# Moving the first hand-over from layer 1 to layer 2 earlier, and layer 2 ahead of layer 1 in unit 12

## The chip, the cores and the metric

One core of one Trainium2 chip. The metric is the device time of one execution of the whole program, in microseconds (us), lower is better. TensorE is PE, ScalarE is ACT, VectorE is DVE, GpSimd is POOL, SyncE is SP.

## The reference

The input x is 2 sequences of 4096 tokens with 192 channels. Three stages follow one another, all in float32:

```python
# 1: causal convolution along the sequence, 7 taps, softmax-normalised weights per head
x = einsum('hk,bskhg->bshg', softmax(weight), windows_of(x))     # (8192, 192)
# 2: "layer 1", a rational activation between two products
h = x @ w_in1                                                     # (8192, 2048)
g = (a0 + a1*h + a2*h**2 + a3*h**3) / (1 + |b0||h| + |b1|h**2 + 1e-6)
x = g @ w_out1                                                    # (8192, 192)
# 3: "layer 2", a squared rectifier between two products
h = x @ w_in2                                                     # (8192, 2048)
y = (s * maximum(h, 0)**2 + b2) @ w_out2                          # (8192, 192)
```

## The kernel before, in words

The tokens are cut into 16 tiles of 512. The 2048 inner features are cut into 8 groups of 256, each two halves of 128 rows. One tile with one group is a **unit**, so there are 128 units for each layer. In the code `n` is layer 1's unit, `t` its tile, `j` its place in the tile, and `m = n - 11` (`SKEW`) is layer 2's unit that is worked on beside it. "Unit 12" below means the pass with n = 12, which holds unit 12 of layer 1 and unit 1 of layer 2.

Every engine runs a program of its own, written out by hand in a fixed order, and engines meet only through counting semaphores. An engine whose next instruction waits does nothing behind it. On each engine the function `phase` is unrolled over all units.

**Layer 1, unit n.** PE's first product (L456 to L460, ten matmuls of 512 columns) writes `h1` in PSUM. The products are split into high and low parts, so each half of the features takes five matmuls. ACT then computes two linear or absolute-value parts of it (`first_steps`, L877 and L878). DVE multiplies them with `h1` in three steps (L1104, L1107, L1110); the last of these signals `t3_done`, after which `h1` may be overwritten. ACT goes on with Abs, Ln and Exp (L954, L969, L882), and one unit later DVE finishes with three last steps (L1136, L1143, L1147), signalling `g_ready`. ACT casts the result to its high part `gh` (L887), POOL subtracts for the low part `gl` (L445), and PE's second product (L469 to L478, ten matmuls) sums them over the eight units of a tile in `o1` and `o1_tail`. This second product trails by three units (`OUT1_LAG`): unit 7 of layer 1 is summed in the pass of unit 10, and unit 8, the first of tile 1, in that of unit 11.

**Hand-over from layer 1 to layer 2.** After the eighth unit of a tile, the sum leaves PSUM. ACT copies the upper half of `o1_tail` to `x2_sum` (L909) and `o1` to `x2_hi` (L910). DVE adds the halves of the tail (L1069, `sum_o1_tail`), casts that (L1074, `round_o1_tail`) and subtracts for `x2_lo` (L1063, `split_o1`). POOL makes the low part of the tail (L420). These stand at the head of the pass with `j == X2_STEP`, which is 3: for tile 0, the pass of unit 11. The next tile may be summed into `o1` only when DVE has read it (L596, L597).

**Layer 2, unit m.** PE's first product (`first_product_of_layer_2`, L487 to L498, ten matmuls) writes `h2`, ACT rectifies it (L914, Relu) in the next pass, squares it later in that pass (L958), and PE's second product (L505, later L665) sums two units behind. `h2` is one buffer: the first product of unit m waits for `u_ready`, the Relu of unit m - 1. At L911 the Relu of unit m - 1 is the first thing that ACT does in pass n; so the Relu of unit 0 stands at the head of pass 12.

**Order on PE.** The passes 0 to 10 take layer 1's first product one unit ahead (`EARLY` is 10), in two buffers. In the passes 11 and 12 (L780 to L819) the order is: first product of layer 1 of that unit (after `t3_done` of the unit before it), first product of layer 2, second product of layer 1. From pass 13 on (`ROWS_FROM`) `unit_by_rows` (L616) takes over, in which the matmuls use half the rows of the array and pairs of them run side by side; its first matmuls (L637) wait for `t3_done` of the unit before (L674), then for `gh` and `gl` (L683, L684).

**Order on ACT** in a pass (L901 to L997): the hand-over if j is 3; Relu of m - 1; copies of the convolution; `first_steps` of n (not for the units 1 to 10, which have had it ahead); cast `gh` of n - 2; Exp of n - 1; in pass 10 a copy of the convolution's tail (L850, called at L951); Abs of n; Square of m - 1; Ln of n, which also waits for `gl` of n - 2; and casts of layer 2's weights (L833; one in pass 11).

**Order on DVE** in a pass (L1089 to L1154): the hand-over if j is 3, the three first steps of n, then the three last steps of n - 1. **POOL** in pass 11: L420, then `gl` of unit 9 (L445).

```python
if unit(n) and not (n <= EARLY):                 # L780
    product_of_layer_1(n, j, t, parity)
...
if unit(m):                                      # L805
    ...
    pe.wait_ge(u_ready, counted(m))
    ...
    first_product_of_layer_2(k2, x2p, t2)
if tile(t) and unit(n - OUT1_LAG):
    second_product_of_layer_1(n, j, t)
```

Of the kernel before, what the change touches and what calls it, by code (L numbers as in the profile page):

```python
# [5 lines left out]
P = 128  # L6
# [14 lines left out]
def counted(count):  # L21

    return max(count, 0)


def conv_rational_relu2_kernel(nc, x_main, x_tail, weight, w_in1, w_out1, a, b, w_in2, w_out2, s, b2, out):
# [5 lines left out]
    TAIL = D - P  # L32
# [47 lines left out]
    with ExitStack() as ctx:  # L80
# [146 lines left out]
        def in_h2(n):  # L227

            return n < EARLY and n % 2 == 1


        def is_unit_1(n):
            return n == 1
# [27 lines left out]
        def unit(n):  # L261
            return 0 <= n < NU

        def tile(t):
            return 0 <= t < TILES
# [4 lines left out]
        def first(t):  # L270
            return t == 0
# [179 lines left out]
        def _(pe):  # L451
# [317 lines left out]
            def phase(n0, t, i, parity):  # L769
                for j in range(UNITS):  # L770
                    n, m = n0 + j, n0 + (j - SKEW)
                    k2 = (j - SKEW) % UNITS
                    t2 = t + (j - SKEW) // UNITS

                    if by_rows(n):
                        unit_by_rows(n, j, t, parity, m, k2, t2)
                        continue

                    early = n < EARLY
                    if unit(n) and not (n <= EARLY):  # L780
                        product_of_layer_1(n, j, t, parity)
                    if early and n == 0:
                        first_product_of_first_unit()
                    if early:
                        product_of_layer_1(n + 1, (n + 1) % UNITS, (n + 1) // UNITS, (n + 1) // UNITS % 2)

                    if tile(t):
                        second_product_of_layer_2(t, j, m, k2)
                    if j == 3 and first(t):
                        pe.wait_ge(ones_ready, 1)  # L790
                        pe.wait_ge(v2_loaded, 16)
                        for f in range(FT):
                            last = pe.matmul(o2[:, 0, 0, 0:D], ones, v2[:, f, :], start=(f == 0),
                                             stop=(f == FT - 1))
                        last.then_inc(colsum_ready, 1)
                    if early:
                        conv_of_unit(n)
                    if not tile(t):

                        if j < OUT1_LAG - 1 and unit(n - OUT1_LAG):  # L800
                            second_product_of_layer_1(n, j, t)
                        second_product_of_layer_2(t, j, m, k2)
                        if j == OUT1_LAG - 2 and unit(n - OUT1_LAG):
                            second_product_of_layer_1(n + 1, j + 1, t)
                    if unit(m):  # L805
                        if k2 == 0:
                            pe.wait_ge(w_hi_ready, 13)
                            pe.wait_ge(w_lo_ready, 14)
                        if m == UNITS // 2:

                            pe.wait_ge(w_hi_ready, 14)
                            pe.wait_ge(w_lo_ready, 18)
                        pe.wait_ge(u_ready, counted(m))
                        if in_h2(n - 1):
                            pe.wait_ge(t3_done, n)
                        x2p = (parity + (j - SKEW) // UNITS) % 2
# [3 lines that stand above are left out]
# [4 lines left out]
        def _(act):  # L824
# [49 lines left out]
            def first_steps(n, h_flat, t_of_n, w_of_n):  # L874

                act.wait_ge(h1_ready, counted(n + 1))
                nc.scalar.activation(t_of_n, h_flat, ACT.Identity, bias=a2, scale=a3).then_inc(t_ready, 1)  # L877
                nc.scalar.activation(w_of_n, h_flat, ACT.Abs, scale=b1_abs).then_inc(w_ready, 1)  # L878
# [16 lines left out]
            def tail_convolved(pair):  # L895
                if pair == 1:
                    act.wait_ge(conv_copied, 3)
                else:
                    act.wait_ge(tail_step, counted(tail_steps(pair)))

            def phase(n0, t, i, parity):  # L901
                for j in range(UNITS):
                    n, m = n0 + j, n0 + (j - SKEW)
                    buf = j % 2
                    if j == X2_STEP and tile(t - 1):
                        act.wait_ge(out1_done, counted(t * UNITS))
                        act.wait_ge(h2_ready, counted((t - 2) * UNITS))
                        act.wait_ge(x2_tail_lo_ready, counted(t - 1))
                        nc.scalar.copy(x2_sum, o1_tail[TAIL:P, :]).then_inc(x2_tmp_ready, 1)  # L909
                        nc.scalar.copy(x2_hi[1 - parity][:, :], o1[:, :]).then_inc(x2_hi_ready, 1)  # L910
                    if unit(m - 1):  # L911
                        act.wait_ge(h2_ready, counted(m))
                        act.wait_ge(g2_ready, counted(m - 1))
                        nc.scalar.activation(u_relu, h2_flat, ACT.Relu).then_inc(u_ready, 1)  # L914
                    if tile(t) and pair_exists(i + 1) and (parity, j) == A_MAIN:
                        convolved(i + 1)
                        act.wait_ge(h1_ready, counted((i + 1) * 2 * UNITS - UNITS))
# [10 lines left out]
                    if unit(n) and not ahead(n):  # L928

                        act.wait_ge(t3_done, counted(n))  # L930
                        first_steps(n, h1_flat, t_buf, w_abs)
                    if first(t) and j == 0:

                        high_of_w1_main(1)
                        high_of_w1_tail(1)
                        first_steps(1, h2_flat, num_buf[1], q_buf[1])
                        high_of_w1_main(2)
                        high_of_w1_tail(2)
# [10 lines left out]
                    if second(t) and j == 2:  # L949
                        act.wait_ge(conv_summed, 5)  # L950
                        copy_of_conv(conv_tail[:, :], 1)  # L951
                    if unit(n):
                        act.wait_ge(z_done, counted(n + 1))
                        nc.scalar.activation(q_buf[buf], q_buf[buf], ACT.Abs).then_inc(q_ready, 1)  # L954
# [47 lines left out]
        def _(dve):  # L1002
# [86 lines left out]
            def phase(n0, t, i, parity):  # L1089
                for j in range(UNITS):  # L1090
                    n = n0 + j
                    buf = j % 2
                    hi, lo, tail = x2_hi[1 - parity], x2_lo[1 - parity], x2_tail[1 - parity]
                    if j == X2_STEP and tile(t - 1):

                        sum_o1_tail(t)
                        round_o1_tail(t, tail)
                        split_o1(t, hi, lo)
# [9 lines left out]
                    if unit(n):  # L1108
                        dve.wait_ge(t2_done, counted(n + 1))
                        nc.vector.scalar_tensor_tensor(num_buf[buf], t_of_n, a1, h_flat, ALU.add,  # L1110
                                                       ALU.mult).then_inc(t3_done, 1)
                    if j == Y_STEP and tile(t - 2):
                        dve.wait_ge(y_stored, counted((t - 2) * 32))
                        if is_last(t - 2):
# [77 lines left out]
```

## Time and profile before

| | |
|---|---|
| median of 3 executions | 1231.98 us |
| lowest, highest | 1231.79, 1232.21 us |
| the profiled execution, its own time | 1233.5 us |
| its span, first to last instruction | 1231.7 us |
| busy shares: PE, DVE, ACT, POOL | 99, 88, 88, 31% |

The profile describes one execution. In its rows, times are us from the start of the span. A row of the timeline gives start, duration, engine, line, operation, what it writes and reads, and in brackets how long the engine had been idle before it and who ended that. "x2" means that two like instructions are merged in a row. A matmul's duration includes filling and draining, so back-to-back matmuls start closer together than they last; the distance between two starts is what one costs. PEclk is the share of full clock that TensorE was granted.

### The profile page before, as it was taken

Reading aid. Unit: us, or ns where it says so; the run is one execution under the profiler, and the core shown is the slowest. Engines: PE = TensorE matmul, PEld = TensorE weight load, DVE = VectorE, ACT = ScalarE, POOL = GpSimd, SP = SyncE. Lnnn points to the kernel's source line nnn. Section 1 sums busy time; section 2 is a strip of 40 time slices with the busy share of each in tenths; the row PEclk is TensorE's granted clock in tenths of the full one; section 3 lists DMA queues with packets and bytes.
Section 4 is the critical chain, followed back from the end, with each engine's and each line's share of the span. In section 5 each row is a group of like instructions: output and inputs, shape, how many; then the busy total and the mean of one; then the engine's idle time right before and its main releaser. Section 6 shows DMA issues by size and latency. Waiting matters only on the chain.

```text
span 1231.7 us, 25449 instructions
## 1 busy us (share of the span) xinstructions
PE 1217.1 (99%) x10848; PEld 1079.9 (88%) x10848; DVE 1079.5 (88%) x957; ACT 1080.4 (88%) x1128; POOL 382.5 (31%) x196
## 2 busy tenths in 40 slices
PE   8998999999999999999999999999999999999999
PEld 5666898999989989898899999889998998989898
DVE  7998899998999989998999989999899998888810
ACT  7998998989888998899989999898998899888843
POOL 3454333233233232232423333233332333232200
PEclk9999999999999999999999999999999999999999
DMA  7100000000000100001000000001000000000000
GB/s 242 50 17 9 2 1 14 2 18 24 14 1 2 40 1 15 1 9 33 1 15 1 14 28 1 14 2 34 7 14 1 2 14 1 15 1 14 2 14 14
DMA packets 14833, 21.64 MB, mean 18 GB/s; under 512 B 1792, under 2 KB 9984, under 8 KB 14592
## 3 DMA queue, kind: packets, MB, share of 16 engines
q1 hardware_dynamic: 14576, 20.01, 5.5%
q8 instruction: 86, 1.41, 0.5%
q14 instruction: 27, 0.22, 0.1%
q10 hardware_dynamic: 144, 0.01, 0.0%
HBM read 13.72 MB, written 6.29 MB: 16 GB/s over the span
## 4 chain that ended last, share of the span: by engine, by line
PE 92%; DVE 5%; issue 1%; ACT 1%; POOL 0%; POOLq 0%; ACTq 0%; DVEq 0%
PE o L665 24%; PE h L643 20%; PE h L637 19%; PE o L649 13%; PE o_tail L655 8%; PE o L505 3%; DVE work L1104 1%; DVE work L1143 1%; DVE work L1136 1%; DVE work L1110 1%; DVE work L1107 1%; PE o L524 0%; PE h L554 0%; PE h L497 0%; PE h L498 0%
## 5 line engine op out<-in xcount | busy, mean ns | idle before, releaser
L445 POOL TENSOR_TENSOR gl<-work,gh 128x1024 fp32r<-128x1024 f32 x126 | 303.8, 2411 | 496.6 <-ACT gh L887 495.3
L665 PE MATMUL o<-v,work 64*128 64x192 f32 x3680 | 340.6, 322 | 0.0
L665 PEld LDWEIGHTS o<-v,work 64*128 64x128 f32 x3680 | 318.2, 186 | 12.5
L877 ACT ACTIVATE work<-h,coef 128x1024 f32<-128x1024 f32 x128 | 154.3, 1205 | 94.5 <-PE h L637 90.3
L1104 DVE SCALAR_TENSOR_TENSOR work<-work,coef,h 128x1024 f32<-128x1024 f32 x128 | 163.8, 1280 | 75.7 <-ACT work L878 74.3
L1147 DVE SCALAR_TENSOR_TENSOR work<-work,coef 128x1024 f32<-128x1024 f32 x128 | 164.5, 1285 | 4.5
L1110 DVE SCALAR_TENSOR_TENSOR work<-work,coef,h 128x1024 f32<-128x1024 f32 x128 | 164.0, 1281 | 4.5
L1136 DVE SCALAR_TENSOR_TENSOR work<-work,coef 128x1024 f32<-128x1024 f32 x128 | 164.1, 1282 | 0.8 <-ACT work L882 0.8
L1143 DVE SCALAR_TENSOR_TENSOR work<-work 128x1024 f32<-128x1024 f32 x128 | 156.8, 1225 | 4.4
L649 PE MATMUL o<-gl,v_hi 64*128 64x512 f32 x460 | 159.6, 387 | 0.0
L914 ACT ACTIVATE work<-h 128x1024 f32<-128x1024 f32 x128 | 130.5, 1019 | 32.1 <-PE h L498 32.1
L655 PE MATMUL o_tail<-gh,v_tail 64*128 64x512 f32 x460 | 158.0, 388 | 0.0
L649 PE MATMUL o<-gh,v_lo 64*128 64x512 f32 x460 | 157.7, 387 | 0.0
L1107 DVE TENSOR_TENSOR work<-work,h 128x1024 f32<-128x1024 f32 x128 | 155.4, 1214 | 0.0
L969 ACT ACTIVATE work<-work,coef 128x1024 f32<-128x1024 f32 x128 | 147.1, 1149 | 5.9 <-POOL gl L445 3.9
L649 PE MATMUL o<-gh,v_hi 64*128 64x512 f32 x460 | 144.1, 393 | 0.0
L878 ACT ACTIVATE work<-h,coef 128x1024 f32<-128x1024 f32 x128 | 142.3, 1111 | 0.0
L655 PE MATMUL o_tail<-gl,v_tail 64*128 64x512 f32 x460 | 141.1, 386 | 0.0
L882 ACT ACTIVATE work<-work 128x1024 f32<-128x1024 f32 x128 | 136.6, 1067 | 0.0
L887 ACT CAST gh<-work 128x1024 fp32r<-128x1024 f32 x128 | 133.8, 1045 | 3.2 <-DVE work L1147 2.9
L958 ACT ACTIVATE work<-work 128x1024 f32<-128x1024 f32 x128 | 135.2, 1056 | 0.3
L954 ACT ACTIVATE work<-work 128x1024 f32<-128x1024 f32 x128 | 135.4, 1058 | 0.0
(142 smaller groups left out, 2696.3 us busy)
## 6 DMA issues: line engine op xcount, KB each, us to landing
out_dram<-y_out SPq DMA_DIRECT2D x32, 192.0 KB, 2.1
xt<-in_x_main_dram SPq DMA_DIRECT2D x7, 518.0 KB, 4.3
xt_tail<-in_x_tail_dram SPq DMA_DIRECT2D x8, 259.0 KB, 4.6
work<-in_moe_w_out_dram SPq DMA_DIRECT2D x2, 768.0 KB, 8.1
v<-in_moe_w_out_dram SPq DMA_DIRECT2D x1, 1536.0 KB, 6.2
raw_w_tail_late<-in_moe_w_in_dram SPq DMA_DIRECT2D x4, 256.0 KB, 6.7
work<-in_moe_w_in_dram SPq DMA_DIRECT2D x2, 512.0 KB, 7.0
xt<-in_x_main_dram SPq DMA_DIRECT2D x2, 259.0 KB, 5.2
```

The costliest lines, as they stand in the source:

```text
L445: nc.gpsimd.tensor_tensor(gl[:, j % 2, :], r_buf[j % 2], gh[:, j % 2, :].bitcast(F32), ALU.subtract).then_inc(gl_ready, 1)
L637: return pe.matmul(h1[:, half, :], weights[rows, c], x[rows, :], start=(upper == (half == 1) and at == 0), stop=(upper != (half == 1) and ...
L643: return pe.matmul(h2[:, half, :], weights[rows, c], x[rows, :], start=(upper == (half == 1) and at == 0), stop=(upper != (half == 1) and ...
L649: return pe.matmul(o1[:, :], weights[rows, 2 * k + half, :], g[rows, buf, half * TOK:(half + 1) * TOK], start=(k == 0 and not upper and at ...
L655: return pe.matmul(o1_tail[:, :], weights, (gh, gl)[at // 2][rows, buf, half * TOK:(half + 1) * TOK], start=(k == 0 and upper and at == 0) ...
L665: last = pe.matmul(o2[:, bank, c, 0:D], g2[buf_out][rows, col:col + P], v2[rows, f, :], start=(f == 0 and c == 0 and turn == 0), stop=(f = ...
L1104: nc.vector.scalar_tensor_tensor(q_buf[buf], w_of_n, b0_abs, h_flat, ALU.add, ALU.mult).then_inc(z_done, 1)
L1107: nc.vector.tensor_tensor(t_of_n, t_of_n, h_flat, ALU.mult).then_inc(t2_done, 1)
L1110: nc.vector.scalar_tensor_tensor(num_buf[buf], t_of_n, a1, h_flat, ALU.add, ALU.mult).then_inc(t3_done, 1)
L1136: nc.vector.scalar_tensor_tensor(q, q, one_eps, r, ALU.add, ALU.mult).then_inc(e_done, 1)
L1143: nc.vector.scalar_tensor_tensor(r, q, 2.0, r, ALU.subtract, ALU.mult, reverse0=True).then_inc(r1_done, 1)
L1147: nc.vector.scalar_tensor_tensor(r, num, a0, r, ALU.add, ALU.mult).then_inc(g_ready, 1)
```

## The change

Four edits, all in the first tile's hand-over:

- ACT's two copies of the hand-over of tile 0 move from the head of pass 11 into pass 10, behind the copy of the convolution's tail and ahead of Abs of unit 10 (`sum_out(1, 0)`).
- DVE's three steps of it move from the head of pass 11 into pass 10, between the three first steps of unit 10 and the three last steps of unit 9.
- The Relu of unit 0 of layer 2 moves from the head of pass 12 into pass 11, behind `first_steps` of unit 11 and ahead of the cast of unit 9.
- In pass 12 PE takes the first product of unit 1 of layer 2 ahead of the first product of unit 12 of layer 1.

The other 15 tiles and all later units keep their order. No instruction is added or removed.

```diff
--- before.py
+++ after.py
@@ -229,6 +229,9 @@
             return n < EARLY and n % 2 == 1
 
 
+        def is_unit_0(n):
+            return n == 0
+
         def is_unit_1(n):
             return n == 1
 
@@ -777,6 +780,10 @@
                         continue
 
                     early = n < EARLY
+                    if is_unit_1(m):
+
+                        pe.wait_ge(u_ready, counted(m))
+                        first_product_of_layer_2(k2, (parity + (j - SKEW) // UNITS) % 2, t2)
                     if unit(n) and not (n <= EARLY):
                         product_of_layer_1(n, j, t, parity)
                     if early and n == 0:
@@ -802,7 +809,7 @@
                         second_product_of_layer_2(t, j, m, k2)
                         if j == OUT1_LAG - 2 and unit(n - OUT1_LAG):
                             second_product_of_layer_1(n + 1, j + 1, t)
-                    if unit(m):
+                    if unit(m) and not is_unit_1(m):
                         if k2 == 0:
                             pe.wait_ge(w_hi_ready, 13)
                             pe.wait_ge(w_lo_ready, 14)
@@ -898,20 +905,27 @@
                 else:
                     act.wait_ge(tail_step, counted(tail_steps(pair)))
 
+            def sum_out(t, of_x2):
+
+                act.wait_ge(out1_done, counted(t * UNITS))
+                act.wait_ge(h2_ready, counted((t - 2) * UNITS))
+                act.wait_ge(x2_tail_lo_ready, counted(t - 1))
+                nc.scalar.copy(x2_sum, o1_tail[TAIL:P, :]).then_inc(x2_tmp_ready, 1)
+                nc.scalar.copy(x2_hi[of_x2][:, :], o1[:, :]).then_inc(x2_hi_ready, 1)
+
+            def relu(m):
+                act.wait_ge(h2_ready, counted(m + 1))
+                act.wait_ge(g2_ready, counted(m))
+                nc.scalar.activation(u_relu, h2_flat, ACT.Relu).then_inc(u_ready, 1)
+
             def phase(n0, t, i, parity):
                 for j in range(UNITS):
                     n, m = n0 + j, n0 + (j - SKEW)
                     buf = j % 2
-                    if j == X2_STEP and tile(t - 1):
-                        act.wait_ge(out1_done, counted(t * UNITS))
-                        act.wait_ge(h2_ready, counted((t - 2) * UNITS))
-                        act.wait_ge(x2_tail_lo_ready, counted(t - 1))
-                        nc.scalar.copy(x2_sum, o1_tail[TAIL:P, :]).then_inc(x2_tmp_ready, 1)
-                        nc.scalar.copy(x2_hi[1 - parity][:, :], o1[:, :]).then_inc(x2_hi_ready, 1)
-                    if unit(m - 1):
-                        act.wait_ge(h2_ready, counted(m))
-                        act.wait_ge(g2_ready, counted(m - 1))
-                        nc.scalar.activation(u_relu, h2_flat, ACT.Relu).then_inc(u_ready, 1)
+                    if j == X2_STEP and tile(t - 1) and not second(t):
+                        sum_out(t, 1 - parity)
+                    if unit(m - 1) and not is_unit_0(m - 1):
+                        relu(m - 1)
                     if tile(t) and pair_exists(i + 1) and (parity, j) == A_MAIN:
                         convolved(i + 1)
                         act.wait_ge(h1_ready, counted((i + 1) * 2 * UNITS - UNITS))
@@ -929,6 +943,9 @@
 
                         act.wait_ge(t3_done, counted(n))
                         first_steps(n, h1_flat, t_buf, w_abs)
+                    if is_unit_0(m):
+
+                        relu(m)
                     if first(t) and j == 0:
 
                         high_of_w1_main(1)
@@ -949,6 +966,7 @@
                     if second(t) and j == 2:
                         act.wait_ge(conv_summed, 5)
                         copy_of_conv(conv_tail[:, :], 1)
+                        sum_out(1, 0)
                     if unit(n):
                         act.wait_ge(z_done, counted(n + 1))
                         nc.scalar.activation(q_buf[buf], q_buf[buf], ACT.Abs).then_inc(q_ready, 1)
@@ -1091,7 +1109,7 @@
                     n = n0 + j
                     buf = j % 2
                     hi, lo, tail = x2_hi[1 - parity], x2_lo[1 - parity], x2_tail[1 - parity]
-                    if j == X2_STEP and tile(t - 1):
+                    if j == X2_STEP and tile(t - 1) and not second(t):
 
                         sum_o1_tail(t)
                         round_o1_tail(t, tail)
@@ -1109,6 +1127,11 @@
                         dve.wait_ge(t2_done, counted(n + 1))
                         nc.vector.scalar_tensor_tensor(num_buf[buf], t_of_n, a1, h_flat, ALU.add,
                                                        ALU.mult).then_inc(t3_done, 1)
+                    if j == X2_STEP - 1 and second(t):
+
+                        sum_o1_tail(t)
+                        round_o1_tail(t, tail)
+                        split_o1(t, hi, lo)
                     if j == Y_STEP and tile(t - 2):
                         dve.wait_ge(y_stored, counted((t - 2) * 32))
                         if is_last(t - 2):
```

## Rows read from the trace of the kernel before

**Rows 1.** The page: the chain that ended last, shares by engine.

```profile
PE 92%; DVE 5%; issue 1%; ACT 1%; POOL 0%; POOLq 0%; ACTq 0%; DVEq 0%
```

**Rows 2.** Waits of PE, whole span: total, times, longest.

```profile
PE h L456 <- POOL w_tail_lo L360: 2.4, 1, 2.4
```

**Rows 3.** Timeline of PE, passes 10 and 11.

```profile
94.82 0.50 PE L456 MATMUL h<-x_hi,w_hi 128*128 128x512 f32 x1 [1.38 <-DVE work L1110]
...
97.01 0.40 PE L460 MATMUL h<-x_tail,w_tail_lo 128*128 128x512 f32 x1
...
100.24 0.73 PE L492 MATMUL h<-x_lo,w_hi 128*128 128x512 f32 x2 [1.58 <-DVE x_lo L1063]
101.16 0.47 PE L497 MATMUL h<-x_tail,w_tail_hi 128*128 128x512 f32 x1 [0.19 <-POOL x_tail L420]
```

**Rows 4.** Timeline of PE, passes 11 to 14.

```profile
102.19 0.63 PE L469 MATMUL o<-gh,v_hi 128*128 128x512 f32 x1
...
105.17 0.56 PE L478 MATMUL o_tail<-gl,v_tail 128*128 128x512 f32 x1
...
106.03 0.39 PE L456 MATMUL h<-x_hi,w_hi 128*128 128x512 f32 x1
...
108.07 0.39 PE L460 MATMUL h<-x_tail,w_tail_lo 128*128 128x512 f32 x1
...
112.60 0.39 PE L478 MATMUL o_tail<-gl,v_tail 128*128 128x512 f32 x1
114.66 0.50 PE L637 MATMUL h<-x_hi,w_hi 64*128 64x512 f32 x2 [1.67 <-DVE work L1110]
...
123.77 0.40 PE L637 MATMUL h<-x_hi,w_hi 64*128 64x512 f32 x2
```

**Rows 5.** Timeline of ACT, passes 10 to 12.

```profile
93.65 1.06 ACT L954 ACTIVATE work<-work 128x1024 f32<-128x1024 f32 x1
...
96.15 0.58 ACT L909 COPY x_sum<-o_tail 64x512 f32<-64x512 f32 x1
...
98.62 1.10 ACT L878 ACTIVATE work<-h,coef 128x1024 f32<-128x1024 f32 x1
...
103.58 1.15 ACT L969 ACTIVATE work<-work,coef 128x1024 f32<-128x1024 f32 x1 [1.03 <-POOL gl L445]
...
105.58 1.02 ACT L914 ACTIVATE work<-h 128x1024 f32<-128x1024 f32 x1
108.56 1.21 ACT L877 ACTIVATE work<-h,coef 128x1024 f32<-128x1024 f32 x1 [1.96 <-PE h L460]
```

**Rows 6.** Timeline of DVE, passes 10 to 12.

```profile
94.68 1.28 DVE L1136 SCALAR_TENSOR_TENSOR work<-work,coef 128x1024 f32<-128x1024 f32 x1
...
98.45 0.68 DVE L1069 TENSOR_TENSOR x_sum<-o_tail,x_sum 64x512 f32<-64x512 f32 x1
...
100.11 1.26 DVE L1104 SCALAR_TENSOR_TENSOR work<-work,coef,h 128x1024 f32<-128x1024 f32 x1
...
102.54 1.28 DVE L1110 SCALAR_TENSOR_TENSOR work<-work,coef,h 128x1024 f32<-128x1024 f32 x1
...
113.32 1.28 DVE L1110 SCALAR_TENSOR_TENSOR work<-work,coef,h 128x1024 f32<-128x1024 f32 x1
```

**Rows 7.** Timeline of POOL, pass 11.

```profile
99.73 1.29 POOL L420 TENSOR_TENSOR x_tail<-x_sum,x_tail 64x512 fp32r<-64x512 f32 x1 [4.85 <-DVE x_tail L1074]
101.09 2.40 POOL L445 TENSOR_TENSOR gl<-work,gh 128x1024 fp32r<-128x1024 f32 x1
```

**Rows 8.** Windows of 3 us: length, busy PE, PEld, DVE, ACT, POOL, PEclk, DMA.

```profile
24.00:27.00 3.00, 3.00 (x8) 2.31 (x8) 2.54 (x3) 2.93 (x4) 3.00 (x3) 0.50 0.73 254
...
99.00:102.00 3.00, 1.57 (x6) 1.04 (x7) 2.96 (x5) 3.00 (x4) 2.19 (x2) 1.00 0.00 0
102.00:105.00 3.00, 3.00 (x9) 2.37 (x8) 2.96 (x3) 1.97 (x3) 1.49 (x1) 0.52 0.02 5
...
114.00:117.00 3.00, 2.34 (x20) 1.96 (x22) 2.97 (x3) 2.51 (x3) 0.17 (x1) 1.00 0.00 0
```

## The prediction

> **What bounds the kernel.** I read the chain that ended last, then PE's waits, then the timeline of each engine around passes 10 to 13. The chain is PE for 92% [rows 1]. PE's waits are few, and the last of any size is the one ahead of pass 13: L637 starts at 114.66 after 1.67 us idle, and pass 14 starts at 123.77, 9.11 later, without a wait [rows 4]. From there to the end PE has a full pass of work for every pass. So the time is "when pass 13 starts" plus a fixed rest, and whatever the change does before 114.66 counts only by how far it moves that start, or by what it makes pass 13 itself cost.
>
> What sets the 114.66? Read it backwards. L637 waits for DVE's third step of unit 12, which runs 113.32 to 114.60 [rows 6]. It hangs on ACT's first step of unit 12, begun at 108.56 after 1.96 us idle [rows 5], and that on PE's first product of unit 12, 106.03 to 108.46 (last matmul 108.07 + 0.39) [rows 4]. So the path is PE's queue up to that product, then 6.2 us of ACT and DVE. In front of it PE loses time in three ways: 1.58 us for `x2_lo`, 0.19 us for the tail's low part [rows 3], and a stretch in which the granted clock was 0.52 of full, the 1.2 GHz level [rows 8], in which a matmul costs 0.426 us ((105.17 - 102.19) / 7) in place of 0.227 us ((108.07 - 106.03) / 9) [rows 4].
>
> **Part by part, for the profiled execution.**
>
> ACT's two copies move to where Abs of unit 10 started, 93.65. They took 1.20 us (L909 at 96.15 and L910 behind it, done at 97.35; I take the difference of that and 96.15) [rows 5]. So `x2_hi` is ready at about 94.85 and not 97.35. Abs and Ln of unit 10 slip by 1.2, to about 96.9, but the next `first_steps` waits for PE's product until 97.5 anyway, so ACT pays nothing.
>
> DVE's three steps cost 1.66 us (98.45 to the next start, 100.11) [rows 6]. They now begin at 94.68, where the last steps of unit 9 began, and end at 96.34. The last steps of unit 9 then run 96.34 to about 100.1, and DVE comes to unit 11 at 100.11 as before: the same work in another order. Unit 11's inputs from ACT are there at 99.72 (98.62 + 1.10) [rows 5]. So the third step of unit 11 still ends at 103.82 (102.54 + 1.28) [rows 6]. What is later is `g` of unit 9, by 1.66 us, to 100.2.
>
> POOL's tail step took 1.29 us [rows 7] and hung on DVE; it now runs from about 95.9 to 97.2.
>
> PE's first product of unit 11 starts at 94.82 as before and its next slot is 97.24 (97.01 + 0.23) [rows 3]. Layer 2's unit 0 follows at once, its inputs being there: ten matmuls, 2.27, to 99.5. Then the second product with k = 0, ten at full clock, to 101.8.
>
> The Relu of unit 0 waits for the former and for `first_steps` of unit 11: about 99.7 to 100.7 (it takes 1.02) [rows 5]. It delays the cast `gh` of unit 9 from 99.6 to 100.75. POOL's `gl` takes 2.40 [rows 7] and now ends near 104.3 rather than 103.5; ACT's Ln of unit 11, which waits for it, goes from 103.58 to 104.4, and the weight cast behind it ends its slot 2.0 later (103.58 to 105.58) [rows 5], at 106.4. The cover of all this is that ACT's next job, `first_steps` of unit 12, comes only after PE's product; without it each of these delays would be paid.
>
> PE in pass 12: layer 2's unit 1 needs the Relu (100.7) and runs 101.8 to 104.05. Layer 1's unit 12 needs 103.82, so the reorder fills the wait with work. It starts at 104.1 in place of 106.03. The gain on the path is thus 1.9 us. As a check: the 8.79 us from 97.24 to 106.03 held 20 matmuls, 4.54 us at full rate, so 4.25 us were stalls and low clock. They go, but ten more matmuls of layer 2, 2.27 us, now stand ahead of the product that matters: 4.25 - 2.27 = 2.0, of which I give 0.05 to waits. Had PE kept its order, DVE's 103.82 would have been the floor, so no more than 2.2 was to be had.
>
> Then `first_steps` of unit 12 starts at 106.65 (ACT free at 106.4), DVE's third step ends at 112.7, and pass 13 could start at 112.75: 1.9 earlier.
>
> **The new idle.** PE's work after layer 1's unit 12 shrinks, as layer 2 is already done. Before, it was busy to 112.99 (112.60 + 0.39) and idle for 1.67 [rows 4]. Now only the second product is left: 104.1 + 20 x 0.227, done at 108.8, and idle until 112.75, some 3.9 us. The rows of this trace show what idle time does to the clock. After 2.4 us idle at one place [rows 2] the clock was 0.50 [rows 8]; after 1.58 and 0.19 us close together it was 0.52; after 1.67 and 1.38 us [rows 3, 4] it stayed 1.00 [rows 8]. 3.9 us is longer than any of them, so I expect pass 13 to begin at the 1.2 GHz level. The price: the low stretch of pass 11 held 8 slow matmuls, 3.4 us, which cost 8 x 0.2 = 1.6 us. Part of the next one may lie in the idle time; I take 1.4, bounds 0.9 and 1.7. PE has no slack in pass 13, so it is paid in full. For this execution the sum is -1.9 + 1.4 = -0.5: 1233.0 against 1233.5.
>
> **Against the runs timed.** The profiled execution is 1.52 us above the median, nearly the 1.6 us that the low stretch of pass 11 costs, and that stretch came after idle time barely longer than others that did nothing. So either the profiler costs 1.5, or the runs timed mostly don't have that stretch. In the second case the second product of pass 11 ends at 102.19 + 2.27 = 104.45, unit 12's product starts there and not at 106.03, and the change gains 0.35 only. That fits the numbers better, and I take it: 1231.98 - 0.35 + 1.4 = 1233.0. The other reading gives 1231.98 - 1.9 + 1.4 = 1231.5. The credit for the removed stretch is the unknown with the widest bounds, 0 to 1.6.
>
> The Trainium skill, "TensorE: Matmul & The Clock Gate", section "What's actually happening", says that the gate's watching is free-running and does not reset when a kernel starts. By that the borderline fall of pass 11 may come in one execution and stay out of the next, while the sum from the rows would be the same; no run here shows it yet.
>
> **Rivals.** What a measurement of this kernel can tell from no change is about 0.2%, 2.46 us.
>
> A. Forecast: low clock at the start of pass 13, 1233.0 (1231.5 if the timed runs had the old stretch). Chance 0.73.
>
> B. The clock holds at 2.4 GHz through the idle. For it: 1.67 us in the same place did nothing. Against: 2.4 us did. Time: 1231.98 - 0.35 = 1231.6, or with the full credit 1230.1. Chance 0.15. The Trainium skill's same page, section "HAM oscillation — how this bites in real kernels", tells that matmul bursts with long idle gaps between them start each burst at the low clock. By that rule pass 13 pays (A); by the row of the same place, 1.67 us and no fall, it does not (B); the gap is new in size, so no row settles it.
>
> C. Slower: the clock stays low for two stretches in place of one, because pass 13 starts too late to raise it. Place: L637 onward. Price 2 x 1.6 = 3.2, so 1231.98 - 0.35 + 3.2 = 1234.8. It decides from 2.8 us of price on. Against it: in pass 11 a single stretch of 3.4 us was enough. Chance 0.06.
>
> D. The hand-over isn't earlier, as ACT's copy waits for PE's last sum of the tile, or ACT's slip of 1.2 reaches `first_steps` of unit 12 (0.25 us of room). Time: within 0.5 of before plus the low clock, 1232 to 1233.9; I put 1233.4. Chance 0.06.
>
> **How the numbers follow.** Forecast 1233.0. A's two readings with their bounds cover 1231.0 to 1233.3, B's first is inside; D adds up to 1233.9, C is mostly left out, and so is B with full credit. Range 1230.7 to 1234.1. Faster by 0.2% means under 1229.5, which only B with full credit and a mistake of 0.6 reaches: 0.04. Slower means over 1234.4: C and a little: 0.06. The rest, 0.9, is no change.
>
> **What would show it.** In the changed profile: L910 near 94.3; L492 without a wait; the second product of pass 11 at 0.227 a matmul; L456 of unit 12 near 104.1; L637 of pass 13 near 112.75 after 3.9 us idle, and PEclk about 0.5 in the slices behind it with pairs of L637 0.43 apart; pass 14 about 10.5 later. If PEclk stays 1.00 there, A is wrong; if L456 of unit 12 starts after 104.6, a wait that I left out is at work.

## The result and the profile after

The changed kernel takes 1234.07 us, median of 21 runs (1232.85 to 1235.13); the kernel before takes 1232.36 us beside it, median of 21 runs (1231.44 to 1233.9). The ratio is 1.0013, with a 95% interval of 1.0007 to 1.0019: slower by 1.7 us, less than the 0.2% that the prediction set as its limit.

The profiled execution took 1234.27 us, its span 1232.5 us. The chain still is PE's:

```profile
PE 92%; DVE 6%; issue 1%; ACT 1%; POOL 0%; POOLq 0%; ACTq 0%; DVEq 0%
```

The longest wait of PE in the changed kernel (total, times, longest). Those for `x2_lo` and the tail's low part are gone, and this one of 3.9 us has come:

```profile
PE h L640 <- DVE work L1128: 3.9, 1, 3.9
```

The timeline of PE, passes 10 to 14; L459 is L456 of before, L490 is L487, L640 is L637:

```profile
94.69 0.50 PE L459 MATMUL h<-x_hi,w_hi 128*128 128x512 f32 x1 [1.65 <-DVE work L1128]
...
97.09 0.39 PE L490 MATMUL h<-x_hi,w_hi 128*128 128x512 f32 x1
...
101.62 0.39 PE L490 MATMUL h<-x_hi,w_hi 128*128 128x512 f32 x1
...
104.48 0.50 PE L459 MATMUL h<-x_hi,w_hi 128*128 128x512 f32 x1 [0.43 <-DVE work L1128]
...
108.92 0.39 PE L481 MATMUL o_tail<-gl,v_tail 128*128 128x512 f32 x1
113.24 0.79 PE L640 MATMUL h<-x_hi,w_hi 64*128 64x512 f32 x2 [3.93 <-DVE work L1128]
113.83 0.62 PE L640 MATMUL h<-x_hi,w_lo 64*128 64x512 f32 x2
114.26 0.63 PE L640 MATMUL h<-x_lo,w_hi 64*128 64x512 f32 x2
...
125.00 0.41 PE L640 MATMUL h<-x_hi,w_hi 64*128 64x512 f32 x2
```

Layer 2's unit 0 follows unit 11's product without a gap (97.09), its unit 1 starts at 101.62, layer 1's product of unit 12 waits 0.43 us for DVE and starts at 104.48. The hand-over works as the change means it to. But then PE is done at 109.31 and idle for 3.93 us, and pass 13 begins with matmul pairs 0.59 and then 0.43 us apart (113.24, 113.83, 114.26) where 0.23 is the full rate. Pass 13 lasts 11.76 us (113.24 to 125.00); before it lasted 9.11 [rows 4].

ACT, DVE and POOL in passes 10 to 12 of the changed kernel:

```profile
94.14 0.58 ACT L914 CAST x_hi<-o 128x512 fp32r<-128x512 f32 x1
...
99.56 1.03 ACT L919 ACTIVATE work<-h 128x1024 f32<-128x1024 f32 x1
...
104.52 1.15 ACT L987 ACTIVATE work<-work,coef 128x1024 f32<-128x1024 f32 x1 [0.74 <-POOL gl L448]
...
107.14 1.21 ACT L884 ACTIVATE work<-h,coef 128x1024 f32<-128x1024 f32 x1 [0.52 <-PE h L463]
```

```profile
94.55 0.68 DVE L1087 TENSOR_TENSOR x_sum<-o_tail,x_sum 64x512 f32<-64x512 f32 x1
...
96.20 2.00 DVE L1159 SCALAR_TENSOR_TENSOR work<-work,coef 128x1024 f32<-128x1024 f32 x1
...
100.70 1.27 DVE L1122 SCALAR_TENSOR_TENSOR work<-work,coef,h 128x1024 f32<-128x1024 f32 x1
...
103.15 1.28 DVE L1128 SCALAR_TENSOR_TENSOR work<-work,coef,h 128x1024 f32<-128x1024 f32 x1
```

```profile
95.83 1.30 POOL L423 TENSOR_TENSOR x_tail<-x_sum,x_tail 64x512 fp32r<-64x512 f32 x1 [1.10 <-DVE x_tail L1092]
```

`x2_hi` is there at 94.72, and Relu of unit 0 runs at 99.56. DVE's first last-step of unit 9 (L1159) took 2.00 us and not 1.28, so unit 11's steps begin at 100.70 and end at 104.43, although this execution runs 0.13 us ahead of that of before.

Windows of 3 us over the start of pass 13 (columns as in rows 8: length, busy PE, PEld, DVE, ACT, POOL, PEclk, DMA):

```profile
109.00:112.00 3.00, 0.31 (x2) 0.00 (x0) 2.51 (x3) 3.00 (x4) 2.20 (x2) 1.00 0.00 0
112.00:115.00 3.00, 1.76 (x8) 1.47 (x10) 2.96 (x3) 3.00 (x4) 0.73 (x1) 0.52 0.00 0
115.00:118.00 3.00, 3.00 (x16) 2.31 (x16) 1.93 (x2) 0.08 (x1) 0.96 (x1) 0.50 0.00 0
118.00:121.00 3.00, 3.00 (x30) 2.69 (x30) 0.28 (x1) 2.59 (x3) 0.32 (x1) 0.84 0.00 0
```

The granted clock was 1.00 for the first part of PE's idle, and about 0.5, the 1.2 GHz level, from about 112 on, when PE was still idle, until some way into the last window.

**Where the time went.** I cut each span in three: the start to unit 11's first product (L456), from there to pass 13, and the rest.

| profiled execution | to L456 | L456 to pass 13 | rest of the span |
|---|---|---|---|
| before | 94.82 | 19.84 | 1117.04 |
| changed | 94.69 | 18.55 | 1119.26 |

The changed kernel gains 1.29 in the middle and loses 2.2 in the rest. The first column differs by up to 1.6 us between profiles of like code (94.24 to 95.82 in all of this study), so single executions are compared by the other two.

### The profile page after: what moved, and what is told of

Its sections match the earlier page's. It is cut to its first block, busy times and chain, and to the rows that moved or that the text cites. A ratio compares the mean times of both kernels' runs of the same rounds, so it can differ in the third digit from the quotient of the medians.

```text
span 1232.5 us, 25449 instructions
## 1 busy us (share of the span) xinstructions
PE 1217.0 (99%) x10848; PEld 1091.2 (89%) x10848; DVE 1080.1 (88%) x957; ACT 1080.2 (88%) x1128; POOL 382.5 (31%) x196
## 4 chain that ended last, share of the span: by engine, by line
PE 92%; DVE 6%; issue 1%; ACT 1%; POOL 0%; POOLq 0%; ACTq 0%; DVEq 0%
PE o L668 24%; PE h L646 20%; PE h L640 19%; PE o L652 14%; PE o_tail L658 8%; PE o L508 3%; DVE work L1122 1%; DVE work L1128 1%; DVE work L1159 1%; DVE work L1125 1%; DVE work L1166 1%; PE o L527 0%; PE h L557 0%; PE h L491 0%; PE h L490 0%
## 5 line engine op out<-in xcount | busy, mean ns | idle before, releaser
L1159 DVE SCALAR_TENSOR_TENSOR work<-work,coef 128x1024 f32<-128x1024 f32 x128 | 164.8, 1287 | 0.8 <-ACT work L889 0.8
```

What stands on the lines that cost most here:

```text
L1159: nc.vector.scalar_tensor_tensor(q, q, one_eps, r, ALU.add, ALU.mult).then_inc(e_done, 1)
```

## The experiments

Ten runs are told below, k1 to k10. "Fill" means extra matmuls into a PSUM bank that is not in use then; they change no result. Two theories stood at first. Theory 1: the loss is the 1.2 GHz level at the start of pass 13, brought by PE's long idle. Theory 2: it is the late DVE steps in pass 11.

**k1: fill ahead of pass 13.**

```diff
+            def keep_busy(count):
+                pe.wait_ge(conv_copied, 3)
+                for _ in range(count):
+                    pe.matmul(conv_bank[0], w1_hi[:, 0:P], x1_hi[0][:, :], start=True, stop=True)
...
+                    if n == ROWS_FROM:
+                        keep_busy(15)
                     if by_rows(n):
```

> The changed kernel with 15 more matmuls on TensorE, into a PSUM bank that nothing uses then, ahead of its wait of pass 13 (3.4 us of the 3.9 us idle). Theory 1 (the loss is the 1.2 GHz level at the start of pass 13, brought by the idle): PEclk stays 1.00 there, pass 13 starts as late as in the changed kernel (18.5 us after the first product of unit 11) but lasts 9.1 us and not 11.8; the median falls by some 2 us below the changed kernel's, to about 1231.9, no slower than before, and the spread between executions shrinks. Theory 2 (the loss is the late start of DVE's steps in pass 11, the 2.00 us step): the median stays near 1234.

Measured: 1232.09 us (11 runs, 1231.02 to 1233.04), ratio to before 0.9996 (0.9987 to 1.0005), where the changed kernel has 1.0013 (1.0007 to 1.0019). The intervals don't meet; the difference is 2.1 us. The timeline of PE and the window behind pass 13's start:

```profile
109.77 3.56 PE L775 MATMUL o<-x_hi,w_hi 128*128 128x512 f32 x15
113.85 0.50 PE L640 MATMUL h<-x_hi,w_hi 64*128 64x512 f32 x2 [0.52 <-DVE work L1135]
114.19 0.39 PE L640 MATMUL h<-x_hi,w_lo 64*128 64x512 f32 x2
...
122.98 0.39 PE L640 MATMUL h<-x_hi,w_hi 64*128 64x512 f32 x2
```

```profile
113.00:116.00 3.00, 2.48 (x20) 1.80 (x20) 2.97 (x3) 2.70 (x3) 0.41 (x1) 1.00 0.00 0
```

From unit 11's product (95.27) to pass 13 it takes 18.58 us, as in the changed kernel, so the fill moved nothing. Pass 13 lasts 9.13 us at a granted clock of 1.00. Theory 1 holds and accounts for the whole loss; theory 2 does not explain it. The spread between executions (2.0 us against 2.3) hardly shrank, which was not expected.

**k9: the changed kernel once more.**

> The changed kernel once more, unaltered, for a second profile and a second set of times. Theory (the idle of 3.9 us ahead of pass 13 brings the 1.2 GHz level in every execution, but its place and length against the work differ): again a low stretch that covers the start of pass 13, of 3.4 or 6.8 us, the time from the first product of unit 11 to pass 13 again 18.5 us, the rest of the span 1.0 to 2.7 us longer than in the run with 15 fills; median 1.2 to 2.2 us above before. Rival (the low stretch of the first profile was chance): PEclk 1.00 at pass 13 and a median near 1232.5.

Measured: 1234.5 us (11 runs), ratio 1.0012 (1.0004 to 1.0021). PE's timeline and the windows of its profile:

```profile
114.18 0.80 PE L640 MATMUL h<-x_hi,w_hi 64*128 64x512 f32 x2 [3.93 <-DVE work L1128]
114.77 0.63 PE L640 MATMUL h<-x_hi,w_lo 64*128 64x512 f32 x2
...
124.86 0.42 PE L640 MATMUL h<-x_hi,w_hi 64*128 64x512 f32 x2
```

```profile
114.00:117.00 3.00, 2.82 (x14) 2.26 (x16) 2.93 (x4) 2.03 (x3) 0.00 (x0) 0.53 0.00 0
117.00:120.00 3.00, 3.00 (x32) 2.71 (x30) 0.90 (x1) 1.36 (x2) 1.28 (x1) 0.91 0.00 0
```

Same idle, 3.93 us, and 18.55 us to pass 13. The low stretch is shorter this time: the clock is back early in the window from 117. Pass 13 lasts 10.68 us, 1.55 more than in k1, where the first profile had 2.63 more. So the fall came in both profiles, and its price was 1.6 in one and 2.6 in the other.

It came in the other executions too. The mean granted clock of a whole execution is on record beside its time: it is 0.999 in the profiles without a low stretch after 30 us (k1), 0.997 with one of some 3.4 us (before, k9) and 0.996 with the one twice as long (changed). All 32 executions of the changed kernel, the first 21 and k9's 11, have 0.995 to 0.997, 18 of them under 0.997, with medians 0.5 (first 21) and 1.2 us (k9) above the rest; k1's 11 have 0.998 or 0.999. The mean doesn't say where in the kernel the clock was low.

**k6: half of the fill.** `keep_busy(8)` in place of 15.

> The changed kernel with 8 more matmuls ahead of the wait of pass 13 in place of 15: some 2.1 us of idle stay. Theory (the loss follows the length of the idle ahead of pass 13): between the changed kernel and the run with 15: idle of 1.6 to 1.8 us brought a fall in some executions of the kernel before, so 1232.3 to 1233.2, nearer to the run with 15 (1232.1). Rival (any fill serves): as with 15.

Measured: 1232.66 us, ratio 1.0002 (0.9993 to 1.0011). In its profile the clock is 1.00 from 30 us to the end, after this idle:

```profile
113.27 0.50 PE L640 MATMUL h<-x_hi,w_hi 64*128 64x512 f32 x2 [2.12 <-DVE work L1135]
```

So 2.1 us of idle brought no fall in the execution that was profiled. The mean clock was 0.997 in two of the 11 executions and 0.998 or 0.999 in nine. The time lies between k1's and the changed kernel's, as expected, but the interval doesn't part it from k1's.

**k5: the kernel before, filled.** k2 had the same two fills, but its first fill also ran in the pass that begins the last tile of layer 2. There it wrote over output sums of the tile before, which were still being added up, and put six matmuls on the path. Its time (1233.4 us) is therefore no measure; up to pass 13 it is the same program as k5. k2's first fill, and k5's, which runs in pass 11 alone:

```diff
+                if k == 0:
+                    pe.wait_ge(conv_copied, 3)
+                    for _ in range(6):
+                        pe.matmul(conv_bank[0], w1_hi[:, 0:P], x1_hi[0][:, :], start=True, stop=True)
```

```diff
+                if k == 0 and first(t2):
+                    pe.wait_ge(conv_copied, 3)
+                    for _ in range(6):
+                        pe.matmul(conv_bank[0], w1_hi[:, 0:P], x1_hi[0][:, :], start=True, stop=True)
                 if k == 0:
                     pe.wait_ge(x2_lo_ready, counted(t2 + 1))
...
+                    if n == ROWS_FROM:
+                        keep_busy(7)
```

> The kernel before, with TensorE kept busy in two of its waits: 6 matmuls ahead of the wait for x2_lo in pass 11, 7 ahead of that of pass 13. It measures what the 1.2 GHz level costs the kernel before. Theory 1 (the low stretch of pass 11 comes in some executions only): the median falls by 0.3 to 0.8 us, the lowest times stay near 1231.4, the high ones (1233.5 and more) thin out. If the profiler alone had made the 1.5 us between the profiled execution and the first median, its own time would stay near 1233.5; by theory 1 it falls to about 1232.

> The kernel before with 6 more matmuls ahead of the wait for x2_lo in pass 11 alone and 7 ahead of that of pass 13, into a PSUM bank that is unused then. Theory (the 1.2 GHz level comes in pass 11 of the kernel before in some executions): no low stretch between 30 us and the end, a median 0.3 to 0.8 us below that of before, the high times thinned out. Rival (the low level isn't what spreads the times): median and spread as before, within 0.2 us.

Measured for k5: 1232.18 us (1231.61 to 1234.19, 11 runs) beside 1232.47, ratio 0.9999 (0.999 to 1.0007). PE's timeline:

```profile
95.81 0.50 PE L456 MATMUL h<-x_hi,w_hi 128*128 128x512 f32 x1 [1.03 <-DVE work L1121]
...
101.49 0.73 PE L496 MATMUL h<-x_lo,w_hi 128*128 128x512 f32 x2 [0.20 <-DVE x_lo L1074]
...
114.32 0.50 PE L641 MATMUL h<-x_hi,w_hi 64*128 64x512 f32 x2
```

No low stretch after 30 us, and 18.51 us from L456 to pass 13 where the profile of before had 19.84. In k2's profile it is 18.27 us (95.40 to 113.67); k5's PE also waited 0.37 us for `x2_hi`. So the low stretch of pass 11 cost that one execution 1.3 to 1.6 us. How often a low stretch comes in other executions their mean clocks tell: of the 81 executions of the kernel before that were timed beside the experiments, 41 have 0.996 or 0.997 and a median of 1232.98 us, the other 40 have 0.998 or 0.999 and 1232.21 (the two values alike); all 11 of k5 have 0.998 or 0.999. So about half of the executions pay some 0.8 us, and the credit of the change is small: k5's median moved by 0.3 us, within the interval. The 18.51 and 18.27 are the numbers to hold against the changed kernel's 18.55: **with the clock out of it, the change gains nothing ahead of pass 13**, and may lose 0.3 us there. The expectation on the profiled execution's own time failed too: it was 1232.99, not near 1232, as this execution reached L456 1.0 us later than that of before.

**k3 and k4: parts of the change.** k3 undoes the fourth edit (PE's order in pass 12); k4 undoes the third as well (Relu of unit 0), which leaves the earlier hand-over alone.

```diff
-                    if is_unit_1(m):
-                        pe.wait_ge(u_ready, counted(m))
-                        first_product_of_layer_2(k2, (parity + (j - SKEW) // UNITS) % 2, t2)
...
-                    if unit(m) and not is_unit_1(m):
+                    if unit(m):
```

and in k4 on ACT also

```diff
-                    if unit(m - 1) and not is_unit_0(m - 1):
+                    if unit(m - 1):
                         relu(m - 1)
...
-                    if is_unit_0(m):
-                        relu(m)
```

> The changed kernel with TensorE's order in pass 12 undone: layer 1's unit 12 first. It waits for DVE until about 104.5, idle for 2.8 us there, and again 1.6 us ahead of pass 13. Theory 1: pass 13 starts as early as in the changed kernel unless the clock falls at 104.5; the 3.9 us idle is cut in two, so the loss is smaller or moved to pass 12: 1232.5 to 1233.8. Theory 2 (DVE's floor makes the loss and the order is worth nothing): 1234.1, as the changed kernel.

> Of the change only the earlier hand-over (ACT's two copies and DVE's three steps); Relu of unit 0 and TensorE's order as before. Theory 1: as the run with the old order, within 0.3 us, as Relu at 105.5 is in time for TensorE at 106.7. Rival: Relu behind the weight cast delays the first steps of unit 12, then 0.5 us and more above the run with the old order. If the 2.00 us of DVE's first last-step of unit 9 is due to the moved Relu, it is 1.28 us here; if it is due to the moved steps of DVE and POOL, it stays 2.00.

Measured: k3 1233.03 us, ratio 1.0004 (0.9995 to 1.0013); k4 1233.18 us, ratio 1.0005 (0.9997 to 1.0014). PE's timeline in k3, then in k4:

```profile
104.02 0.60 PE L459 MATMUL h<-x_hi,w_hi 128*128 128x512 f32 x1 [2.64 <-DVE work L1124]
104.41 0.63 PE L460 MATMUL h<-x_lo,w_hi 128*128 128x512 f32 x1
...
114.35 0.50 PE L640 MATMUL h<-x_hi,w_hi 64*128 64x512 f32 x2 [1.65 <-DVE work L1124]
```

```profile
105.21 0.50 PE L459 MATMUL h<-x_hi,w_hi 128*128 128x512 f32 x1 [2.65 <-DVE work L1121]
...
108.26 0.50 PE L490 MATMUL h<-x_hi,w_hi 128*128 128x512 f32 x1 [0.49 <-ACT work L915]
...
114.19 0.50 PE L640 MATMUL h<-x_hi,w_hi 64*128 64x512 f32 x2 [1.10 <-DVE work L1121]
```

ACT in k4:

```profile
107.19 1.02 ACT L915 ACTIVATE work<-h 128x1024 f32<-128x1024 f32 x1
108.11 1.20 ACT L880 ACTIVATE work<-h,coef 128x1024 f32<-128x1024 f32 x1
```

In k3 the idle is cut in two, 2.64 and 1.65 us. In this profile the clock fell right after the first, and most of the ten matmuls of unit 12's product were 0.43 apart; pass 13 came 20.11 us after L456. In k4, with the same first idle (2.65), it did not fall, and pass 13 came after 18.76 us. The 0.2 us more than the changed kernel's 18.55 lie on ACT: its Relu of unit 0 (L915) stands ahead of the first steps of unit 12 (L880), which start 2.90 us after unit 12's product does (108.11 - 105.21) and not 2.66 (107.14 - 104.48). So an idle of 2.65 us brings the fall in one execution and not in another. By the mean clocks k4's profile is of the rarer kind: nine of its 11 executions have 0.997, and nine of k3's have 0.997 or less. Both times are where theory 1 put them, and both kernels seem to cost less than the change as a whole, but the intervals overlap. The moved Relu is not what slows DVE's step: that took 1.99 us in k4 too.

**k10: the old order with both waits filled.** On top of k3, with `keep_busy(7)` ahead of pass 13:

```diff
                     if unit(n) and not (n <= EARLY):
+                        if is_unit_1(m):
+                            keep_busy(11)
                         product_of_layer_1(n, j, t, parity)
```

> The changed kernel with TensorE's old order in pass 12 and both of its waits filled: 11 more matmuls ahead of layer 1's product of unit 12, 7 ahead of pass 13. It asks what the new order is worth once the clock is out of it. Theory (DVE's third step of unit 11 sets when layer 1's product of unit 12 starts, in either order): 18.5 to 18.7 us from the first product of unit 11 to pass 13, no low stretch after 30 us, and the median of the run with 15 fills, 1232.1, within 0.4 us. Rival (the order gains by itself): 0.5 us and more above it.

Measured: 1232.53 us, ratio 0.9997 (0.9988 to 1.0006), k1's being 0.9996. The intervals of k9 and k1 just touch (1.0004, 1.0005), but k10 was timed beside k9, and its slowest execution (1233.14) is below the fastest of k9's (1233.21).

```profile
95.82 0.50 PE L459 MATMUL h<-x_hi,w_hi 128*128 128x512 f32 x1 [1.70 <-DVE work L1133]
...
102.75 2.65 PE L775 MATMUL o<-x_hi,w_hi 128*128 128x512 f32 x11
105.60 0.50 PE L459 MATMUL h<-x_hi,w_hi 128*128 128x512 f32 x1 [0.19 <-DVE work L1133]
...
114.36 0.50 PE L640 MATMUL h<-x_hi,w_hi 64*128 64x512 f32 x2
```

18.54 us from L456 to pass 13 (114.36 - 95.82) against k1's 18.58. The fourth edit, which made the long idle, gains nothing by itself: in either order unit 12's product waits for DVE (0.19 us here, 0.43 in the changed kernel).

**k7: POOL's tail step parted from DVE's.** All of k1, and in pass 11:

```diff
                         pool.wait_ge(x2_tail_hi_ready, counted(t))
+                        if second(t):
+                            pool.wait_ge(g_ready, 10)
```

> The changed kernel with 15 fill matmuls ahead of pass 13, in which POOL's step on the tail (L420 in the kernel before) also waits until DVE has ended the last step of unit 9. It parts POOL's step from DVE's first last-step of unit 9, which took 2.00 us in place of 1.28 in four profiles with the moved steps. Theory (DVE's step, which reads two operands in SBUF, can't start while POOL's runs; DVE's steps with one operand in PSUM can): it takes 1.28 us again, and unit 11's first DVE step comes 0.7 us earlier after the first product of unit 11. By the Trainium skill, SBUF — State Buffer, the pair of ports that the two share is locked for a whole instruction, which would give the same. Rival (the step is slow for another reason, such as the moved steps themselves): 2.00 us stays. TensorE waits longer for the tail's low part, so the time isn't the point.

DVE's timeline, POOL's, and PE's wait in pass 11:

```profile
95.97 1.27 DVE L1168 SCALAR_TENSOR_TENSOR work<-work,coef 128x1024 f32<-128x1024 f32 x1
...
99.73 1.28 DVE L1131 SCALAR_TENSOR_TENSOR work<-work,coef,h 128x1024 f32<-128x1024 f32 x1
...
106.43 2.64 DVE L1168 SCALAR_TENSOR_TENSOR work<-work,coef 128x1024 f32<-128x1024 f32 x1 [2.98 <-ACT work L898]
```

```profile
99.98 1.26 POOL L425 TENSOR_TENSOR x_tail<-x_sum,x_tail 64x512 fp32r<-64x512 f32 x1 [5.42 <-DVE work L1179]
105.58 2.41 POOL L450 TENSOR_TENSOR gl<-work,gh 128x1024 fp32r<-128x1024 f32 x1 [4.33 <-ACT gh L903]
```

```profile
101.39 0.77 PE L502 MATMUL h<-x_tail,w_tail_hi 128*128 128x512 f32 x1 [2.98 <-POOL x_tail L425]
```

The step took 1.27 us, and unit 11's first DVE step came 5.28 us after L456 (94.45) where the changed kernel has 6.01 (100.70 - 94.69): 0.73 earlier, as expected. The run shows the reverse as well. POOL's `gl` now runs from 105.58 to 107.99 and meets DVE's same step of unit 10, begun at 106.43: it took 2.64. In both cases DVE ends 1.07 or 1.08 us after POOL does (98.20 and 97.13; 109.07 and 107.99), as if it began just before POOL's end. At 99.98 POOL's step ran beside L1131, which reads one operand from PSUM, and that took its usual 1.28. The Trainium skill, "SBUF — State Buffer", section "SBUF: two separate sides", says that a DVE step with two SBUF inputs and a POOL step that reads SBUF exclude each other for a whole instruction; the runs agree. The time, 1235.66 us in the one execution there is, is no measure of the step: PE waits 2.98 us for the tail in pass 11, and the granted clock fell behind that wait (0.50 from 102 to 103.5).

**k8: DVE makes the tail's low part itself,** on top of k1.

```diff
                         split_o1(t, hi, lo)
+                        dve.wait_ge(x2_tail_hi_ready, 1)
+                        nc.vector.tensor_tensor(tail[TAIL:P, :], x2_sum, tail[0:TAIL, :].bitcast(F32),
+                                                ALU.subtract).then_inc(x2_tail_lo_ready, 1)
```

> The changed kernel with 15 fill matmuls ahead of pass 13, in which DVE itself makes the tail's low part of tile 0 behind split_o1 and POOL does not. Theory (POOL's step holds DVE's up by 0.72 us): the first last-step of unit 9 takes 1.28 us, DVE pays 0.4 to 0.7 us for the added step, so unit 11's steps come 0 to 0.3 us earlier than in the run with 15 fills, and the median is 1231.8 to 1232.1. Rival: the step stays at 2.00 us and the median goes up by 0.5 us.

```profile
96.29 0.69 DVE L1144 TENSOR_TENSOR x_tail<-x_sum,x_tail 64x512 fp32r<-64x512 f32 x1
97.01 1.28 DVE L1170 SCALAR_TENSOR_TENSOR work<-work,coef 128x1024 f32<-128x1024 f32 x1
...
100.79 1.28 DVE L1130 SCALAR_TENSOR_TENSOR work<-work,coef,h 128x1024 f32<-128x1024 f32 x1
```

Measured: 1232.42 us, ratio 1.0 (0.9991 to 1.0009). The step is back at 1.28, but the added one costs 0.72 (96.29 to 97.01), so unit 11's steps start 6.12 us after L456 (94.67), no earlier than the 6.01 of the changed kernel. The contention was shown again and its cure is worth nothing. Two parts of the expectation missed: the start 0 to 0.3 us earlier, and the median of 1231.8 to 1232.1.

## Why the prediction was right, and where its terms were off

The forecast was 1233.0 in a range of 1230.7 to 1234.1, "no change" with 0.9; measured are 1234.07 and a ratio of 1.0013. The direction and the mechanism (rival A) held. The time lies 0.03 us inside the upper bound, and that it did not fall outside is luck: two terms were mis-sized, both the same way, so the change cost 1.7 us where the forecast had 1.0. The forecast also built on a median of three executions, 1231.98, that became 1232.36 over 21.

- **What bounds the kernel**: held. Without a low stretch the rest of the span behind pass 13's start was 1116.6 to 1117.2 us in nine profiles. Only how far that start moves, and what pass 13 costs, counted.
- **"ACT pays nothing"**: held; `x2_hi` at 94.72, unit 12's first step at 107.14 after 0.52 us idle.
- **"The last steps of unit 9 then run 96.34 to about 100.1, and DVE comes to unit 11 at 100.11 as before: the same work in another order"**: failed. The order brought L1159 beside POOL's tail step, where it took 2.00 us: 0.72 more, not in any row that I had used. The rows of before showed POOL's step beside DVE steps that read PSUM only [rows 6, 7]. So unit 12's product started 9.79 us after L456 and not 9.3, and pass 13 after 18.55 and not 17.9.
- **The gain of 0.35 us for the runs timed**: came out at zero or below, 18.55 against 18.51 in k5 and 18.27 in k2, for the same reason. The 18.27 is what the forecast took for the kernel before without its low stretch (114.66 - 1.58 - 94.82 = 18.26), so the miss lies in the changed kernel. The 1.9 us for the profiled execution came out at 1.29.
- **The new idle of 3.9 us and the low clock behind it**: held in place and length (3.93 us, clock 0.52 and 0.50). k1 shows that it is the cause of the loss.
- **The price, "I take 1.4, bounds 0.9 and 1.7"**: the term with the largest error. Pass 13 was longer than k1's by 2.63 us in one profile and 1.55 in the other, and the medians say 2.1. I had sized it by one stretch of 3.4 us, the length of that of pass 11. In the first profile the low level covered two such lengths, begun before PE had work again, so that it was only partly worked at. This is what rival C described. Its price of 3.2 was too high; the longer stretch itself was no rarity, as 18 of the 32 executions of the changed kernel have a mean clock like that profile's or lower.
- **"Either the profiler costs 1.5, or the runs timed mostly don't have that stretch"**: the dilemma was incomplete. The low stretch cost that execution 1.3 to 1.6 us (19.84 against 18.51 and 18.27), and the way to L456 differs by up to 1.6 us from one execution to the next besides. The second half, "mostly don't have that stretch", was too strong: about half of the executions have a low mean clock (k5).
- **Rival B** (the clock holds): refuted by both profiles and by the mean clock of all 32 executions. Rival D: its waits on ACT did not come, yet PE did wait 0.43 us, on DVE.

The sum with measured terms is 0 to +0.3 for the start of pass 13 and +1.6 to +2.6 for its clock. About half of the executions of the kernel before pay some 0.8 us for a low stretch of their own (k5), which takes 0.4 off the difference. The measured +1.7 lies in what is left, +1.2 to +2.5.

No version beat the kernel before by more than its interval. The best were k1 (0.9996), k10 (0.9997) and k5 (0.9999).

## What to carry to other kernels

A reorder that gathers an engine's work early gathers its idle time too: ask where the freed time will lie as one piece, and on TensorE price what follows it at half the clock, at up to twice the length of a low stretch seen elsewhere. When a step moves, look up not only its duration but also what runs beside it in its new place: a DVE step with both inputs in SBUF beside a POOL step costs most of the overlap (0.72 of 0.93 us, 1.36 of 1.56). And before crediting a removed stall, check whether the profiled execution is a typical one; here the mean granted clock of every execution told it.

## What the runs showed of the hardware that was not expected

- Idle of 1.67 us [rows 4], 2.12 (k6) and 2.65 (k4) was followed by a granted clock of 1.00; 1.58 and 0.19 close together [rows 3, 8], 2.64 (k3), 2.98 (k7), 3.93 (changed) and 3.93 (k9) by about 0.5. Nearly the same gap, 2.64 and 2.65 us, did both, so a gap's length alone does not decide in one execution. Over the executions the fall gets more frequent with it: by the mean clock two of 11 with 2.12 us (k6), nine of 11 with 2.65 us (k4), 32 of 32 with 3.93 us.
- The same program with the same gap got 6.8 us of low clock in one profile (three windows of 3 us at 0.52, 0.50 and 0.84: 3.4 us of clock lost, so 6.8 at half) and half of that in the other (0.53 and 0.91).
- DVE's scalar_tensor_tensor on two SBUF operands ended 1.07 to 1.08 us after the POOL step it met, in two different overlaps (0.93 and 1.56 us), while one with a PSUM operand beside a POOL step took its usual 1.28.
